# Second group's attention on TensorE: turns by batches and q's products by heads, as row tiles of 64 rows that write two PSUM banks

## The reference, cut to what matters

```python
kv = einsum('bhsd,bhse->bhde', k, v)            # batch 4, heads 8, seq 576, head_dim 64
o = einsum('bhsd,bhde->bhse', q, kv)
o = o / sqrt(mean(o * o, -1) + 1e-6) * g_norm
x = o with heads side by side                   # 2304 tokens x 512
h = x @ w_in;  x = (h * sigmoid(h)) @ w_out     # d_ff 2048
out = (x @ w_a * (x @ w_b)) @ w_out2            # d_ff 1536
```

## Time and profile before

| | |
|---|---|
| median of 3 runs | 897.32 us (896.08 to 897.57) |
| profiled execution, time | 897.5 us |
| profiled execution, span of its records | 895.7 us |
| TensorE busy | 868.0 us, 97% of the span |
| VectorE, ScalarE, GpSimd busy | 520.8, 282.0, 626.3 us |
| TensorE's granted clock | 0.999 of full |

### The profile page before, as it was taken

How to read it: one execution, slowest core, us unless ns; L and a number is a source line. 1 busy time by engine, 2 the same in 40 slices (tenths; PEclk the granted TensorE clock), 3 DMA queues, 4 the chain that set the end, 5 groups by cost and what they waited for, 6 DMA issues and landing times.

```text
span 895.7 us, 16996 instructions
## 1 busy us (share of the span) xinstructions
PE 868.0 (97%) x6582; PEld 821.9 (92%) x6582; DVE 520.8 (58%) x816; ACT 282.0 (31%) x470; POOL 626.3 (70%) x911
## 2 busy tenths in 40 slices
PE   7889999999999999999999999999999999999998
PEld 6678899999999999999989999999998999999996
DVE  2697575657887665556774454453573544545536
ACT  2764353434543322222432121121251221211210
POOL 1596446654597777775588687887979877777760
PEclk9999999999999999999999999999999999999999
DMA  9742232510011111111111011111110250111103
GB/s 269 177 101 75 67 62 56 120 47 26 27 45 48 48 49 48 49 48 48 33 40 48 25 48 50 46 48 48 48 48 25 84 140 24 52 48 44 48 25 106
DMA packets 47103, 55.63 MB, mean 62 GB/s; under 512 B 11952, under 2 KB 32432, under 8 KB 47024
## 3 DMA queue, kind: packets, MB, share of 16 engines
q1 hardware_dynamic: 44304, 49.55, 20.1%
q10 hardware_dynamic: 2720, 4.98, 1.9%
HBM read 49.81 MB, written 4.72 MB: 61 GB/s over the span
## 4 chain that ended last, share of the span: by engine, by line
PE 86%; DVE 7%; POOL 2%; issue 2%; ACT 1%; DMA 1%; SPq 0%; DVEq 0%; ACTq 0%; POOLq 0%
PE ps L734 45%; PE ps L798 7%; PE ps L799 7%; PE ps L800 7%; PE ps L820 5%; PE ps L822 5%; PE ps L821 5%; PE ps L691 2%; DVE x_lo L1290 2%; DMA kvq<-in_v_dram 1%; PE ps L665 1%; PE ps L701 1%; DVE g_lo L1358 1%; DVE o_sb L1249 1%; DVE ps L1336 1%
## 5 line engine op out<-in xcount | busy, mean ns | idle before, releaser
L734 PE MATMUL ps<-x_hi,w_hi 128*128 128x288 f32 x1092 | 236.5, 298 | 4.8 <-ACT kept L1038 2.4
L734 PE MATMUL ps<-x_lo,w_hi 128*128 128x288 f32 x1092 | 234.0, 296 | 0.0
L734 PE MATMUL ps<-x_hi,w_lo 128*128 128x288 f32 x1092 | 232.9, 295 | 0.0
L734 PEld LDWEIGHTS ps<-x_hi,w_hi 128*128 128x128 f32 x1092 | 179.1, 188 | 17.1 <-POOL w_lo L478 5.0
L734 PEld LDWEIGHTS ps<-x_hi,w_lo 128*128 128x128 f32 x1092 | 176.1, 189 | 0.0
L734 PEld LDWEIGHTS ps<-x_lo,w_hi 128*128 128x128 f32 x1092 | 174.7, 188 | 0.0
L476 POOL TENSOR_SCALAR w_hi<-wt 128x256 fp32r<-128x256 f32 x156 | 70.4, 451 | 129.4 <-PE ps L734 125.1
L798 PE MATMUL ps<-g_hi,d_hi 128*128 128x288 f32 x512 | 154.2, 301 | 3.2 <-DVE g_lo L1358 1.2
L1038 ACT COPY kept<-ps 128x576 f32<-128x576 f32 x117 | 75.1, 642 | 254.2 <-PE ps L734 253.4
L1372 DVE TENSOR_TENSOR xy<-xy,ps 128x288 f32<-128x288 f32 x224 | 100.8, 453 | 88.5 <-PE ps L800 87.5
L800 PE MATMUL ps<-g_hi,d_lo 128*128 128x288 f32 x512 | 150.9, 295 | 0.0
(11 more groups left out here) (104 smaller groups left out, 1211.4 us busy)
## 6 DMA issues: line engine op xcount, KB each, us to landing
raw<-in_moe_w_out_dram SPq DMA_DIRECT2D x28, 512.0 KB, 3.8
raw<-in_moe_w_in_dram SPq DMA_DIRECT2D x15, 512.0 KB, 3.5
raw<-in_moe_w_a_dram SPq DMA_DIRECT2D x12, 512.0 KB, 3.6
raw<-in_moe_w_b_dram SPq DMA_DIRECT2D x12, 512.0 KB, 3.5
kvq<-in_k_dram SPq DMA_DIRECT2D x12, 288.0 KB, 5.1
kvq<-in_v_dram SPq DMA_DIRECT2D x12, 288.0 KB, 6.6
out_dram<-xy SPq DMA_DIRECT2D x27, 128.0 KB, 2.4
kvq<-in_q_dram SPq DMA_DIRECT2D x16, 144.0 KB, 6.4
```

What stands on the lines that cost most here:

```text
L734: mm = pe.matmul(ps[:, bank + s, 0:PART], w, x[:, n, c, s * PART:(s + 1) * PART], start=(begins and first), stop=last, skip_group_check=no ...
```

## The change

All slots of the second group but slots 7 and 8 now take both of the last banks. A turn slot becomes six transposes of 64 rows (one batch each) by 64 moving columns: batch 0's go to BANK_D, batch 1's to BANK_D + 1. A `q_kv` slot becomes twelve products of 64 rows by 64 columns over 64 moving columns, one for each head and batch, without the zero blocks of `kv_sb`: even heads to BANK_D, odd heads to BANK_D + 1. ScalarE's evictions read the same number of elements, 384 in a row, from the two banks, and `o_keep` and `square` put heads back in their old order. The functions of the first group keep their work.

```diff
-    SLOT_BANKS = (2, 1, 1, 1, 1, 1, 1, 0, 0, 1, 1, 1)
+    SLOT_BANKS = (2, 2, 2, 2, 2, 2, 2, 0, 0, 2, 2, 2)
...
+        def slot_banks():
+            return ps[:, BANK_D:BANK_D + 2, 0:TILE3 // 2]
...
+        def by_heads(t):
+            return t.rearrange("p (t h e) -> p h t e", h=2, e=HD)
...
+            def turn_batches(src):
+                for n in range(3):
+                    for bb in range(2):
+                        rows = slice(bb * HALF, (bb + 1) * HALF)
+                        mm = pe.transpose(ps[:, BANK_D + bb, n * HALF:(n + 1) * HALF], src(n)[rows], ident[rows, rows])
+                return mm
+
+            def take_slot(sem, count):
+                wait_turn(BANK_D)
+                wait_turn(BANK_D + 1)
+                turn[BANK_D] = turn[BANK_D + 1] = (sem, count)
+
+            def q_turn1(h, j):
+                i = UNITS + JS * h + j
+                pe.wait_ge(q_in[0], 32 + 64 * (h + 1))
+                take_slot(qT_kept, i + 1)
+                turn_batches(lambda n: by_tiles(1, h, 3 * j + n)).then_inc(qT_mm, 1)
+
+            def q_kv1(h, j):
+                i = UNITS + JS * h + j
+                pe.wait_ge(qT_kept, i + 1)
+                pe.wait_ge(kv_kept, PAIRS + h + 1)
+                take_slot(o_kept, i + 1 - UNITS)
+                for n in range(3):
+                    for odd in range(2):
+                        rows = slice(odd * HALF, (odd + 1) * HALF)
+                        for bb in range(2):
+                            at = bb * TILE3 // 2 + n * HALF
+                            mm = pe.matmul(ps[bb * HALF:(bb + 1) * HALF, BANK_D + odd, n * HD:(n + 1) * HD],
+                                           qT_sb[rows, i % 3, at:at + HALF], kv_sb[rows, h % 2, bb, rows],
+                                           start=True, stop=True)
+                mm.then_inc(o_mm, 1)
+
+            def o_turn1(h, j):
+                i = UNITS + JS * h + j
+                pe.wait_ge(n_ready, i + 1)
+                take_slot(x_kept, i + 1)
+                turn_batches(lambda n: o_sb[:, i % 3, n * P:(n + 1) * P]).then_inc(oT_mm, 1)
...
-                nc.scalar.copy(o_sb[:, i % 3, :], ps[:, bank, 0:TILE3]).then_inc(o_kept, 1)
+                nc.scalar.copy(by_heads(o_sb[:, i % 3, :]),
+                               slot_banks().rearrange("p h (t e) -> p h t e", e=HD)).then_inc(o_kept, 1)
...
-                nc.scalar.copy(qT_sb[:, i % 3, :], ps[:, bank, 0:TILE3]).then_inc(qT_kept, 1)
+                nc.scalar.copy(qT_sb[:, i % 3, :].rearrange("p (m n) -> p m n", m=2), slot_banks()).then_inc(qT_kept, 1)
```

More of the change, by code:

```diff
@@ L306, in staged @@
             return (0, h + 2) if G else (h, 1)
-        slot_turn, tile_turn, turns = [], [], 0
+        tile_turn, turns = [], 0
         for pp in range(PAIR0[-1] + 1):
@@ L313, in fused_attention_ffn_kernel @@
             for n in range(steps):
-                slot_turn.append(turns)
                 at = STEPS * pp + n
@@ L325, in tile_bank @@
             return BANK_D + tile_turn[t] % 2
-        def slot_bank(at):
-            return BANK_D + slot_turn[at] % 2
+        def slot_banks():
+            return ps[:, BANK_D:BANK_D + 2, 0:TILE3 // 2]
         def first_bank(h, j):
@@ L669, in kv, with q_turn, q_kv @@
                 turn[b0] = turn[b1] = (kv_kept, PAIRS * G + h + 1)
[L671 to L676, removed]
+            def q_turn(h, j, bank):
+                i = JS * h + j
+                pe.wait_ge(q_ready, i + 1)
                 wait_turn(bank)
                 for n in range(3):
-                    mm = pe.transpose(ps[:, bank, n * P:(n + 1) * P], by_tiles(G, h, 3 * j + n), ident[:])
+                    mm = pe.transpose(ps[:, bank, n * P:(n + 1) * P], by_tiles(0, h, 3 * j + n), ident[:])
                 mm.then_inc(qT_mm, 1)
                 turn[bank] = (qT_kept, i + 1)
-            def q_kv(G, h, j, bank):
-                i = UNITS * G + JS * h + j
+            def q_kv(h, j, bank):
+                i = JS * h + j
                 pe.wait_ge(qT_kept, i + 1)
-                pe.wait_ge(kv_kept, PAIRS * G + h + 1)
+                pe.wait_ge(kv_kept, h + 1)
                 wait_turn(bank)
@@ L693, in q_kv, with o_turn @@
                 mm.then_inc(o_mm, 1)
-                turn[bank] = (o_kept, i + 1 - UNITS) if G else (n_ready, i + 1)
-            def o_turn(G, h, j, bank):
-                i = UNITS * G + JS * h + j
+                turn[bank] = (n_ready, i + 1)
+            def o_turn(h, j, bank):
+                i = JS * h + j
                 pe.wait_ge(n_ready, i + 1)
@@ L712, in attend @@
                 elif a <= 3:
-                    q_turn(1, h, a - 1, slot_bank(at))
+                    q_turn1(h, a - 1)
                 elif a <= 6:
-                    q_kv(1, h, a - 4, slot_bank(at))
+                    q_kv1(h, a - 4)
                 elif a >= 9:
-                    o_turn(1, h, a - 9, slot_bank(at))
+                    o_turn1(h, a - 9)
             def step(u, n):
@@ L899, in _ @@
             for j in range(JS):
-                q_turn(0, 0, j, first_bank(0, j))
+                q_turn(0, j, first_bank(0, j))
             kv(0, 0)
@@ L904, in _ @@
                     if h:
-                        o_turn(0, h - 1, j, first_bank(h - 1, j))
-                    q_kv(0, h, j, first_bank(h, j))
+                        o_turn(h - 1, j, first_bank(h - 1, j))
+                    q_kv(h, j, first_bank(h, j))
                 if h + 1 < PAIRS:
@@ L910, in _ @@
                     for j in range(JS):
-                        q_turn(0, h + 1, j, first_bank(h + 1, j))
+                        q_turn(h + 1, j, first_bank(h + 1, j))
             pe.wait_ge(x_kept, UNITS - JS)
@@ L915, in _ @@
             for j, bank in enumerate((2, 6, 7)):
-                o_turn(0, 3, j, bank)
+                o_turn(3, j, bank)
             pe.wait_ge(n_ready, UNITS)
@@ L931, in _, with square @@
         def _(act):
-            def square(G, h, j, bank):
+            def square(G, h, j, bank=None):
                 i = UNITS * G + JS * h + j
@@ L936, in square, with o_keep @@
                     act.wait_ge(ssq, i if G or j == 0 else i - 1)
[L937 to L942, removed]
+                dst, src = squares(G, j)[:], ps[:, bank, 0:TILE3] if G == 0 else None
+                if G:
+                    dst, src = by_heads(dst), slot_banks().rearrange("p h (t e) -> p h t e", e=HD)
+                nc.scalar.activation(dst, src, ACT.Square).then_inc(sq_ready, 1)
+            def o_keep(h, j):
+                i = UNITS + JS * h + j
+                act.wait_ge(oT_mm, i - 2)
                 if i == UNITS:
                     act.wait_ge(n_ready, UNITS)
-                nc.scalar.copy(o_sb[:, i % 3, :], ps[:, bank, 0:TILE3]).then_inc(o_kept, 1)
+                nc.scalar.copy(by_heads(o_sb[:, i % 3, :]),
+                               slot_banks().rearrange("p h (t e) -> p h t e", e=HD)).then_inc(o_kept, 1)
             def root(G, h):
@@ L950, in root, with keep @@
                                      bias=eps_col[:, 0:1], scale=1.0 / HD).then_inc(rms, 1)
-            def keep(G, h, j, bank):
+            def keep(G, h, j, bank=None):
                 i = UNITS * G + JS * h + j
@@ L957, in keep @@
                 dst = xy[:, G, h * GTOK:(h + 1) * GTOK].rearrange("p (m n e) -> p m n e", m=2, e=HALF)
-                nc.scalar.activation(dst[:, :, 3 * j:3 * j + 3, :],
-                                     ps[:, bank, 0:TILE3].rearrange("p (n m e) -> p m n e", m=2, e=HALF),
-                                     ACT.Copy, scale=gcol[:, 0:1]).then_inc(x_kept, 1)
+                if G:
+                    src = slot_banks().rearrange("p m (n e) -> p m n e", e=HALF)
+                else:
+                    src = ps[:, bank, 0:TILE3].rearrange("p (n m e) -> p m n e", m=2, e=HALF)
+                nc.scalar.activation(dst[:, :, 3 * j:3 * j + 3, :], src, ACT.Copy, scale=gcol[:, 0:1]).then_inc(x_kept, 1)
             def kv_keep(G, h):
@@ L972, in kv_keep, with qT_keep @@
                 cp.then_inc(kv_kept, 1)
-            def qT_keep(G, h, j, bank):
-                i = UNITS * G + JS * h + j
+            def qT_keep(h, j):
+                i = UNITS + JS * h + j
                 act.wait_ge(qT_mm, i + 1)
                 act.wait_ge(o_mm, i - 2)
-                nc.scalar.copy(qT_sb[:, i % 3, :], ps[:, bank, 0:TILE3]).then_inc(qT_kept, 1)
+                nc.scalar.copy(qT_sb[:, i % 3, :].rearrange("p (m n) -> p m n", m=2), slot_banks()).then_inc(qT_kept, 1)
             def attend(at, evict):
@@ L990, in attend @@
                 elif a <= 3:
-                    qT_keep(1, h, a - 1, slot_bank(at))
+                    qT_keep(h, a - 1)
                 elif a <= 6:
-                    square(1, h, a - 4, slot_bank(at))
-                    o_keep(1, h, a - 4, slot_bank(at))
+                    square(1, h, a - 4)
+                    o_keep(h, a - 4)
                 elif a >= 9:
```

(2 more changed lines are left out.)

## The result

The changed kernel takes 905.35 us (median of 5 runs, 904.37 to 907.93) beside 897.57 us for the kernel before in the same comparison: ratio 1.0098, 95% interval 1.0081 to 1.0114. It is slower by 7.3 to 10.2 us, 8.8 in the middle; forecast were +7.4 us and 904.8. The profiled execution took 904.37 us.

What follows compares the result with a forecast made beforehand. TensorE, busy in 97% of the span, was taken to bound the kernel. Ordinary turns 2.6, late flushes 1.3, late evictions 3.4, q_kv 0 and first pair 0.1 gave +7.4 us, 904.8; range 899.5 to 909.5.

Steps and rivals of the forecast that it cites:

- turn slots without late eviction: Second group: 13 ordinary turn slots 0.20 us dearer each, 2.6; three with late flushes 0.42 each, 1.3.
- late flushes: Three o_turn slots (84.07, 127.47, 228.37) must wait for VectorE's second flush, 0.37 us later; growth 0.42 each, 1.3 together.
- late evictions: Five turn slots that ScalarE empties late; the first down tile behind must now wait too, 3.4 us together.
- q_kv slots of pairs 1 and later: Nine slots, each 0.30 us cheaper but followed by 0.31 us of wait, sum 0.
- first pair: Slot 6 comes about 1 us later, but TensorE waits there for VectorE anyway; 0.1 us added.
- The signs: Expected in the trace: 216 more records, slots costing 0.53 and 0.70, nine waits of 0.2 to 0.3 us, five longer.
- The slots: Turn slot 0.53 us instead of 0.33; q_kv slot 0.70 instead of 1.00; both include 0.35 for the tile shape.
- rival B: At turn slots, row tiles of 64x128 pay no drain: +6.1 us, 903.4; chance 0.18.
- Rival C: The two halves of a turn don't run together, 0.18 us more in 16 slots: +10.2, 907.5; chance 0.09.
- wait for the second read: Behind each q_kv slot the down tile waits 0.31 us for ScalarE's second read, the slot's whole gain.
- Rivals D and E: D: half the added delay ends in TensorE's waits, 900.8, chance 0.13; E: waits a quarter real, 894.4, chance 0.10.
- Rival F: ScalarE's reads get longer by 0.11 us each: +9.4 to +10.5, 907.3; chance 0.07.

Runs made afterwards that it cites:

- second profile of before: The kernel before, unchanged, profiled a second time: ratio 0.9994 (0.9980 to 1.0008).
- waits-alone kernel: Kernel before with its own products and one bank written, but second-group slots except 7 and 8 wait for and hold both last banks: 908.1 us, ratio 1.0135.
- early-freed banks: ScalarE copies o to o_sb first and squares the copy, freeing both banks after one read: ratio 0.9996 with only q_kv slots changed, 1.0074 on the changed kernel.
- q_kv-only kernel with early-freed banks: Kernel before with only q_kv slots changed to 64x64 products in both banks, and ScalarE copying o before squaring from o_sb: 895.95 us, ratio 0.9996.
- faster version: Kernel before with q_kv by heads only in pairs of heads 2 to 4, squares from o_sb, eviction ahead of the sixth step's g_hi copy: 895.05 us, ratio 0.9975.
- both remedies: Changed kernel with squares from o_sb and the eviction ahead of the g_hi copy at the sixth step: 901.96 us, ratio 1.0055.
- early-freed banks on the whole change: Changed kernel, but ScalarE copies o to o_sb first and squares from o_sb: 903.52 us, ratio 1.0074.

## Why the prediction was right, point by point

Against the second profile of before, up to the down tile behind the last slot, the changed kernel stands 8.55 us later. By the steps of the prediction:

| term | predicted | in the trace |
|---|---|---|
| turn slots without late eviction (16), late flushes included | 2.6 + 1.3 = 3.9 | 3.5 |
| late evictions (5) | 3.4 | 2.8 |
| q_kv slots of pairs 1 and later (9) | 0 | 0.8 |
| first pair | 0.1 | 0 |
| lower clock behind the wait at 127 us | not foreseen | 1.5 |

The signs came in part. The records and the slots' costs are as said. The waits are there, but the list of waits shows them smaller than I wrote, since it counts from the end of the last record, the way through the pipeline included: none of the nine ordinary ones behind the o_sb copy, and for the five late evictions 0.84, 0.94 and three of 0.2 to 0.4. They are read from the starts.

*The slots.* 0.53 and 0.70 us came out to the hundredth. That a tile of 64 rows by 128 columns pays the same 0.35 us as the two shapes in the earlier trace rows was the open choice, and rival B (no drain) falls with it: the x_lo pair is 0.53 later, where B wanted at most 0.26. The Trainium skill's page "TensorEngine Tiling (Array Packing)", Key Properties, says that a change of tiling mode drains TensorE, with 64x128 among the modes, and the trace now agrees for this shape too, with the 0.35. Rival C falls as well: with halves one after the other the last record would start some 0.35 after the first, not 0.18, and the slot would cost 0.70.

*The waits.* The q_kv slot's gain was eaten by the wait for the second read, as the waits-alone kernel (0.30 to 0.31 a slot) and the early-freed banks show from both sides. Ordinary q_kv slots came out between 0.00 and 0.13. The missing 0.4 is one slot at the sixth step of a pair, whose eviction stands behind the g_hi copy like the late turns'. I had looked for late evictions among turn slots only.

*Late flushes and late evictions* were each priced a little high. The slot at 127 paid its 0.38 (0.37 said), while the two others added only the 0.2 us of an ordinary turn slot. The late evictions came to 0.38, 0.46, 0.67, 0.67 and 0.63: the first two together 0.84 where I had 1.08. Perhaps VectorE's own lateness took up more there than the 0.5 I had taken off; no run separates this.

*The clock* is the term that the sum lacked. Without it the trace would give 7.0, with it 8.55; the timed middle is 8.8. That the forecast of 904.8 is so near the median of 905.35 is in part luck: turn terms too high by 1.0 hid some of the 2.3 us of q_kv slots and clock that the sum did not have, and the two medians are only 7.8 us apart where the interval's middle is 8.8. Rivals D and E (waits taken up) are out: TensorE's waits after the first pair pass on what is put before them nearly in full. Rival F is out too: the copy by heads takes 0.47 us as before.

What stays open: why the q_kv-only kernel with early-freed banks is 2 us ahead in the trace and not in the timed runs. My guess is that its first pair waits more (two waits for o_sb's copy, 0.9 us each), and that the clock falls there in some executions. Its own profile has no such fall. Of the four other kernels in which ScalarE copies first, three have one (clock 0.94 over 46 to 75 us; the faster version has none), but the waits-alone kernel, which squares first, has one too. The mean granted clock of its timed runs is that of before (0.9943 and 0.9941), which does not support the guess. The faster version, which leaves the products and banks of the first pair alone, gives the 2 us; but it differs in the ScalarE order as well, so this is only argued, and its interval overlaps the q_kv-only kernel's.

## What to carry to other kernels

A smaller product is not a cheaper slot: a short burst in another tile shape pays for going in and out, here 0.35 us, so it only helps where the burst saves more than that or where the slot pays it already, as q_kv did. Before you let a burst take both banks of a ping-pong pair, follow both hand-overs, the flush ahead of it and the eviction behind it; if they are longer than the work between them, every slot stalls. Then look at which engine's fixed order the eviction stands in, and free the banks with the first read (0.3 us a slot in the traces here).

## What the runs showed of the hardware

A wait of TensorE can have a cost beyond its length. Behind 1.85 us of waiting the granted clock went to 1.2 GHz for some 3.4 us in 5 of 7 profiles and cost 1.4 to 1.5 us each time (pairs 0.48 us apart in place of 0.265); behind 1.48 us at the same place it never did in 6. The same happens in the kernel before at a wait of 1.9 us for GpSimd near 676 us, in its second profile but not in its first, TensorE's timeline:

```profile
676.42 0.66 PE L734 MATMUL ps<-x_hi,w_hi 128*128 128x288 f32 x2 [1.89 <-POOL w_lo L478]
676.87 0.68 PE L734 MATMUL ps<-x_lo,w_hi 128*128 128x288 f32 x2
```

Over the 13 profiles that wait, 1.85 to 1.91 us in all, was followed by the lower clock in 7. The length of one wait does not decide it, then, and there is no limit between 1.48 and 1.85 us either: in the first pair the clock fell in 4 of the 13 profiles, and in two of these (both remedies, and early-freed banks on the whole change) the longest wait in the 10 us before was 1.45 us. In the changed kernel the same 1.45 us at 57.35 were followed by no fall. What else it takes is open.

Part of the spread between runs of one kernel (894.1 to 899.7 us for before in one comparison) can come from this; how much is not shown. It also means that a single pair of profiles can mislead by 1.5 us, as can the first pair's 1.6 us; the second profile of before settled more than another variant would have.
